# Second raw tiles for queries and keys in the first chunk of an attention and mixture kernel, with a new order of its steps

## The chip, the cores and the metric

The kernel runs on one core of one Trainium2 chip. The metric is the device time of one execution in microseconds (us), as the median of several runs. Engines are named as the profile names them: PE is TensorE, DVE is VectorE, ACT is ScalarE, POOL is GpSimd, and SP is the engine whose queue issues nearly all DMAs.

## The reference

What is computed, cut to what matters (4 batches, 8 heads, 576 positions, head size 64; then 2304 tokens of 512 features and 4 experts with 1024 hidden features, all float32):

```python
scores = (1 / sqrt(64)) * q @ k.T                      # per batch and head
thresh = max(scores) - tau                             # per row
scores = where(scores >= thresh, scores, -1e9)
attn = exp(scores - max(scores)); attn /= sum(attn) + 1e-9
x = attn @ v                                           # heads side by side: (2304, 512)
p = domain_probs / (sum(domain_probs) + 1e-9)          # (2304, 4)
for e in range(4):
    out += p[:, e:e+1] * (relu(x @ w1[e]) @ w2[e])
```

## The kernel before

**Values in two parts.** Products keep nearly full float32 precision by splitting a value into a rounded high part and a low remainder: ACT copies the raw tile to the high part (`q_hi`, `k_hi`, `v_hi`, `whi`, `hhi`), and DVE or POOL subtracts that from the raw tile for the low part (`q_lo`, `k_lo`, `v_lo`, `wlo`, `hlo`). One product is then two or three matmuls.

**Attention.** Two heads form a pair, and each head of a pair and a stretch of queries is a turn. Turns are counted through the kernel. A turn's transposed queries and keys are loaded into `q_raw` and `k_raw`, one tile each, from which the split parts go to tiles that alternate by turn (`q_hl`, `k_hh`, `k_ll`). A unit is 128 query rows of a pair (one unit may hold the end of the first head and the start of the second): `s` on PE makes its scores, then `max` (DVE, L991), `thr`, `exp` (ACT, L904), `mask` (DVE, L1002), `rec` (DVE), `norm` (POOL, L748), `tr` (PE transposes, L794), `phi` (ACT, L911 or L915) and, outside the first chunk, `plo` (DVE, L1014 and L1019) follow, and `pv` or `pv32` on PE multiplies by the values. `x_hi` (ACT) and `x_lo` (POOL) or `x_lo32` (DVE, L1031) split the result, which is the input of the experts.

**Chunks.** Tokens go in five chunks, of 384, 512, 384, 512 and 512. The first chunk has 4 pairs, 8 turns (0 to 7) of 384 queries and 24 units (`LONE` and `SOLID` are both 24). No expert works while they run, and so they may use a second score slot in the experts' PSUM tile `e_ps` (even units use `s_ps`, odd ones `e_ps`), and tiles named `solid` and a third `p` lie in SBUF where the experts' hidden tiles `h_hi` and `h_lo` are later. From unit 24 on units are interleaved with the experts of the chunk before; they have one score slot. The experts work in groups: `up` (PE, L848 to L850), whose result `hhi` (ACT, L940) and `hlo` (DVE, L1042) split, and `down` (PE, L863 to L865), whose result `acc` (DVE) adds up. Weights come in 320 pieces through a stage of 4 tiles into a ring of 14 (`w_load`, `whi` L950, `wlo` on POOL L760 or `wlo_dve` on DVE L1036). 16 pieces make an expert. Of the first expert pieces, those with m % 4 == 2 go to DVE.

**The order.** All engines walk one list, `ORDER`, and each picks its own steps from it, so each engine's instructions have a fixed order and only semaphores move them in time. `timeline()` gives every step a due time. A unit u of the first chunk starts at `first + period * u`, and each of its steps is due at an offset from the table `ALONE`; the later units have a start spread over the expert work and offsets from `AMONG`. The experts' start is `first + 24 * period + experts`. `settle()` then plays the steps through with a fixed duration for each. Whenever an engine is free in this model it takes, of the steps whose conditions in `follows()` are met, the one that is due first; steps of one kind keep their order; an SP step counts as landed 2.4 after its issue, which takes 1.2 (0.6 for a weight piece). Due times are thus priorities, not starting times.

**Loads.** For turn 1 and on, SP's `k_load` (L679) waits until `k_lo` of the turn before has read `k_raw` (`sp.wait_ge(s_klo, turn)`), and `q_load` (L671) until `q_lo` of the turn before has read `q_raw`. `v32_load` (L687, L689) and `v_load` (L695, L698) bring values, L709 weights. `k_lo` of turn 0 is on DVE (`k_lo_dve`, L977), all others on POOL (L733); `q_lo` is on DVE (L972).

Of the kernel before, what the change touches and what calls it, by code (L numbers as in the profile page):

```python
# [5 lines left out]
F32 = mybir.dt.float32  # L6
# [197 lines left out]
def ups_through(t, f):  # L204
# [7 lines left out]
ALONE = dict(load=-9.58, q_hi=6.24, q_lo=16.9, k_hi=3.19, k_lo=-5.05, v_hi=7.8, v_lo=-7.05, max=7.48, thr=16.58,  # L212
             exp=9.73, mask=14.89, eps=11.82, rec=0.41, norm=25.81, tr=-3.84, phi=12.87, plo=8.73, pv=18.85,
             xo=23.42, xs=7.11, x_hi=0.71, x_lo=7.48)
AMONG = dict(load=-9.73, q_hi=2.13, q_lo=6.73, k_hi=-6.56, k_lo=-8.85, v_hi=-5.72, v_lo=7.39, max=-2.85, thr=-2.6,
             exp=8.58, mask=2.91, eps=-2.89, rec=7.65, norm=-1.63, tr=10.81, phi=8.04, plo=-0.34, pv=12.11, xo=4.75,
             xs=15.23, x_hi=9.65, x_lo=8.74)
PLAN = dict(first=3.59, period=2.76, experts=17.92, end=13.35, weights=35.63, weight=8.82, prob=19.0)
# [144 lines left out]
def follows(name, x, half=2):  # L363
# [6 lines left out]
    if name == "k_load":  # L370
        return [(k_low(x - 1), x - 1)] if x else []
    if name in ("q_load", "v_load"):
        return [(name[0] + "_lo", x - 1)] if x else []
# [70 lines left out]
    return [("acc", x)]  # L444

# [80 lines left out]
def build(nc, qT, kT, v, tau, dp, w1, w2, out):  # L526
    ctx = ExitStack()
    with ctx:
# [28 lines left out]
        with nc.sbuf_tensor("solid", [P, FT, PAD], F32) as solid, nc.sbuf_tensor("p2", [P, PAD], F32) as p2:  # L557
            p.append(p2)
# [11 lines left out]
        e_ps = ctx.enter_context(nc.psum_tensor("e_ps", [P, 2, 512], F32))  # L570

# [13 lines left out]
        def head(turn):  # L585
            pair = PAIRS[turn // 2]
            return pair.b * H + 2 * pair.k + turn % 2

# [26 lines left out]
        s_q_ld = sem("s_q_ld")  # L615
        s_k_ld = sem("s_k_ld")
# [39 lines left out]
        TURNS32 = 2 * SOLID_PAIRS  # L656

        @block.sync
        def _(sp):
            sp.dma_start(tau_col[:, 0:1], tau.to_broadcast([P, 1])).then_inc(s_tau_ld, 16)  # L660
            for half in range(2):
                sp.dma_start(q_raw[half * HD:(half + 1) * HD, 0:PAIRS[0].n], qT[0][:, 0:PAIRS[0].n]).then_inc(s_q_ld, 16)
            for name, x in ORDER:
                if name == "q_load":
# [418 lines left out]
```

## Time and profile before

| | us |
|---|---|
| median of 3 runs (1089.19 to 1090.68) | 1090.0 |
| the profiled execution, its own time | 1088.7 |
| its span in the trace | 1086.7 |
| PE busy | 1061.0 (98%) |
| DVE busy | 674.6 (62%) |
| POOL busy | 629.0 (58%) |
| ACT busy | 562.2 (52%) |

The span is that of the profiled execution; its own time is 2.0 us longer, which lies around the span. Times in the trace are counted from the span's start. "Busy" is the time in which an engine executes an instruction; an idle time is put down to the one whose result came last. The granted clock of PE is at full speed in all 40 slices of the page. The chain that ended last is 92% PE, and the page has expert matmuls as its largest lines.

### The profile page before, as it was taken

The numbers are of one execution on the slowest core, as the hardware profiler recorded it, in microseconds if no ns is written. First come the engines' busy times: TensorE is split into PE (matmuls) and PEld (weight loads), VectorE is DVE, ScalarE is ACT, GpSimd is POOL, SyncE is SP. The second block draws the span as 40 slices with busy tenths as digits, with TensorE's granted clock in tenths as the row PEclk, the third lists the DMA queues.
The fourth block names the chain that finished last, engine by engine and source line by source line (L and its number), as shares of the span: only waits on it lengthen the run. The fifth ranks groups of instructions, "written<-read, shape, count | busy, mean of one in ns | idle before, by whom it ended". The sixth has DMA issues, their size and how long they took to land.

```text
span 1086.7 us, 17018 instructions
## 1 busy us (share of the span) xinstructions
PE 1061.0 (98%) x5752; PEld 931.5 (86%) x5752; DVE 674.6 (62%) x1505; ACT 562.2 (52%) x990; POOL 629.0 (58%) x659
## 2 busy tenths in 40 slices
PE   5899999999999999999999999999999999999998
PEld 5789899899888888888899999988888888888887
DVE  6988788787887788777777878752122133343331
ACT  6776566666766647566475656644233232242330
POOL 6756576767886748667486867656444342232220
PEclk9999999999999999999999999999999999999999
DMA  6534344445544424223333433333333244233311
GB/s 163 155 111 123 87 123 133 131 128 156 148 148 120 137 57 121 92 85 115 103 124 111 127 115 116 90 100 123 94 110 88 72 123 136 87 107 97 107 58 39
DMA packets 96788, 121.08 MB, mean 111 GB/s; under 512 B 41152, under 2 KB 45248, under 8 KB 96704
## 3 DMA queue, kind: packets, MB, share of 16 engines
q1 hardware_dynamic: 96400, 119.68, 37.0%
q8 instruction: 47, 0.77, 0.3%
q10 hardware_dynamic: 304, 0.33, 0.1%
q14 instruction: 37, 0.30, 0.1%
HBM read 115.25 MB, written 4.72 MB: 110 GB/s over the span
## 4 chain that ended last, share of the span: by engine, by line
PE 92%; DVE 4%; issue 1%; ACT 1%; POOL 1%; DMA 1%; SPq 0%; ACTq 0%; DVEq 0%
PE e_ps L863 12%; PE e_ps L865 12%; PE e_ps L864 12%; PE e_ps L848 12%; PE e_ps L850 12%; PE e_ps L849 12%; PE t_ps L794 6%; PE s_ps L782 3%; PE x_ps L821 3%; PE s_ps L783 3%; PE x_ps L823 3%; PE x_ps L806 1%; DVE p L1002 1%; DVE small L991 1%; DVE q_hl L972 0%
## 5 line engine op out<-in xcount | busy, mean ns | idle before, releaser
L760 POOL TENSOR_TENSOR w_lo<-stage,w_hi 128x512 fp32r<-128x512 f32 x272 | 355.8, 1319 | 275.6 <-ACT w_hi L950 275.3
L950 ACT ACTIVATE w_hi<-stage 128x512 fp32r<-128x512 f32 x320 | 194.1, 625 | 177.3 <-PE e_ps L865 120.6
L848 PE MATMUL e_ps<-x_hi,w_hi 128*128 128x512 f32 (+1 forms) x640 | 241.3, 377 | 0.2 <-DVE h_lo L1042 0.2
L850 PE MATMUL e_ps<-x_hi,w_lo 128*128 128x512 f32 (+1 forms) x640 | 236.2, 369 | 0.0
L849 PE MATMUL e_ps<-x_lo,w_hi 128*128 128x512 f32 (+1 forms) x640 | 235.8, 368 | 0.0
L863 PE MATMUL e_ps<-w_hi,h_hi 128*128 128x512 f32 x576 | 229.8, 399 | 0.0
L865 PE MATMUL e_ps<-w_hi,h_lo 128*128 128x512 f32 x576 | 225.2, 391 | 0.0
L864 PE MATMUL e_ps<-w_lo,h_hi 128*128 128x512 f32 x576 | 224.8, 390 | 0.0
L1042 DVE SCALAR_TENSOR_TENSOR h_lo<-e_ps,h_hi 128x512 fp32r<-128x512 f32 (+1 forms) x160 | 101.8, 636 | 127.1 <-ACT h_hi L940 125.1
L940 ACT ACTIVATE h_hi<-e_ps 128x512 fp32r<-128x512 f32 (+1 forms) x160 | 88.6, 554 | 118.0 <-PE e_ps L850 117.2
L904 ACT ACTIVATE p<-s_ps,small 128x576 f32<-128x576 f32 x132 | 97.4, 738 | 73.2 <-DVE small L991 72.7
L850 PEld LDWEIGHTS e_ps<-x_hi,w_lo 128*128 128x128 f32 x640 | 120.1, 188 | 15.6
L848 PEld LDWEIGHTS e_ps<-x_hi,w_hi 128*128 128x128 f32 x640 | 120.3, 188 | 13.7 <-DVE h_lo L1042 0.4
L849 PEld LDWEIGHTS e_ps<-x_lo,w_hi 128*128 128x128 f32 x640 | 120.4, 188 | 13.3
L865 PEld LDWEIGHTS e_ps<-w_hi,h_lo 128*128 128x128 f32 x576 | 108.1, 188 | 23.8
L864 PEld LDWEIGHTS e_ps<-w_lo,h_hi 128*128 128x128 f32 x576 | 108.4, 188 | 18.6
L1002 DVE SCALAR_TENSOR_TENSOR p<-s_ps,small,p 128x576 f32<-128x576 f32 x132 | 107.7, 816 | 26.4 <-ACT p L904 22.9
L863 PEld LDWEIGHTS e_ps<-w_hi,h_hi 128*128 128x128 f32 x576 | 108.3, 188 | 18.5
L748 POOL TENSOR_SCALAR p<-p,small 128x576 f32<-128x576 f32 x144 | 110.6, 769 | 22.9 <-DVE small L1009 11.5
L991 DVE TENSOR_REDUCE small<-s_ps 128x1 f32<-128x576 f32 x132 | 99.7, 756 | 34.2 <-PE s_ps L783 32.6
L915 ACT ACTIVATE pt_hi<-t_ps 128x640 fp32r<-128x640 f32 x120 | 84.4, 703 | 53.5 <-PE t_ps L794 52.2
L1059 DVE SCALAR_TENSOR_TENSOR acc<-e_ps,prob,acc 128x512 f32<-128x512 f32 x54 | 40.5, 750 | 111.2 <-PE e_ps L865 110.8
(64 smaller groups left out, 1465.0 us busy)
## 6 DMA issues: line engine op xcount, KB each, us to landing
stage<-w SPq DMA_DIRECT2D x320, 256.0 KB, 2.9
k_raw<-kT SPq DMA_DIRECT2D x94, 144.0 KB, 2.8
v_raw<-v SPq DMA_DIRECT2D x40, 128.0 KB, 2.2
out<-acc SPq DMA_DIRECT2D x18, 256.0 KB, 2.0
q_raw<-qT SPq DMA_DIRECT2D x32, 144.0 KB, 2.9
q_raw<-qT SPq DMA_DIRECT2D x16, 96.0 KB, 2.6
v_raw<-v SPq DMA_DIRECT2D x80, 16.0 KB, 2.1
q_raw<-qT SPq DMA_DIRECT2D x16, 80.0 KB, 2.4
```

The source lines that it names most:

```text
L748: gp.tensor_scalar(tile, tile, col(total, u), 1.0, ALU.mult, ALU.mult).then_inc(s_norm, 1)
L760: gp.tensor_tensor(w_lo[:, m % RING, :], stage[:, m % STAGES, :], w_hi[:, m % RING, :], ALU.subtract).then_inc(s_wl, 1)
L848: mm(ps[:, 0:n], w_hi[:, piece, tile], x_hi[:, k, cols], start=k == 0, stop=False)
L849: mm(ps[:, 0:n], w_hi[:, piece, tile], x_lo[:, k, cols], start=False, stop=False)
L850: op = mm(ps[:, 0:n], w_lo[:, piece, tile], x_hi[:, k, cols], start=False, stop=k == KT - 1)
L863: mm(ps, h_hi[:, f, tile], w_hi[:, piece, :], start=f == 0, stop=False)
L864: mm(ps, h_hi[:, f, tile], w_lo[:, piece, :], start=False, stop=False)
L865: op = mm(ps, h_lo[:, f, tile], w_hi[:, piece, :], start=False, stop=f == FT - 1)
L950: run(w_hi[:, m % RING, :], stage[:, m % STAGES, :], copy).then_inc(s_wh, 1)
L991: ve.tensor_reduce(col(neg_m, u), s_slot(u), AX.XY, ALU.max, negate=True).then_inc(s_max, 1)
L1002: ve.scalar_tensor_tensor(out=tile, in0=s_slot(u), scalar=col(thr, u), in1=tile, op0=ALU.is_ge, op1=ALU.mult, accum_out=col(total, u)).the ...
L1042: ve.scalar_tensor_tensor(out=h_lo[:, g.j, c0:c0 + n], in0=e_ps[:, g.bank, 0:n], scalar=0.0, in1=h_hi[:, g.j, c0:c0 + n], op0=ALU.max, op1 ...
```

## The change

For the 8 turns of the first chunk the raw queries and keys alternate between two tiles each: even turns keep `q_raw` and `k_raw`, odd turns use `q_raw2` (384 columns) and `k_raw2` (576 columns), which lie behind `solid` and the third `p` in the place of `h_hi` and `h_lo`. A load then waits for the low part of two turns before (`raw_before`); turn 8 follows turn 6, and from turn 9 on it is the turn before again. Each of the two load semaphores becomes a pair, one for even and one for odd turns. POOL's `k_lo` of turn 1 gets a wait for `k_lo` of turn 0, which is on DVE, so that the count of `s_klo` keeps its order. All due times are new (`ALONE`, `AMONG`, `PLAN`), and with them the order of all steps.

```diff
@@ -209,13 +209,13 @@
 
 
 
-ALONE = dict(load=-9.58, q_hi=6.24, q_lo=16.9, k_hi=3.19, k_lo=-5.05, v_hi=7.8, v_lo=-7.05, max=7.48, thr=16.58,
-             exp=9.73, mask=14.89, eps=11.82, rec=0.41, norm=25.81, tr=-3.84, phi=12.87, plo=8.73, pv=18.85,
-             xo=23.42, xs=7.11, x_hi=0.71, x_lo=7.48)
-AMONG = dict(load=-9.73, q_hi=2.13, q_lo=6.73, k_hi=-6.56, k_lo=-8.85, v_hi=-5.72, v_lo=7.39, max=-2.85, thr=-2.6,
-             exp=8.58, mask=2.91, eps=-2.89, rec=7.65, norm=-1.63, tr=10.81, phi=8.04, plo=-0.34, pv=12.11, xo=4.75,
-             xs=15.23, x_hi=9.65, x_lo=8.74)
-PLAN = dict(first=3.59, period=2.76, experts=17.92, end=13.35, weights=35.63, weight=8.82, prob=19.0)
+ALONE = dict(load=-11.01, q_hi=5.5, q_lo=23.24, k_hi=9.14, k_lo=-5.05, v_hi=7.26, v_lo=0.26, max=12.61, thr=24.24,
+             exp=16.27, mask=15.64, eps=1.79, rec=3.18, norm=27.13, tr=-0.14, phi=18.57, plo=6.84, pv=25.95,
+             xo=29.77, xs=12.98, x_hi=-1.84, x_lo=4.04)
+AMONG = dict(load=-4.47, q_hi=3.5, q_lo=7.9, k_hi=-3.85, k_lo=-2.77, v_hi=-4.59, v_lo=7.73, max=-4.35, thr=-4.57,
+             exp=8.78, mask=-0.65, eps=-0.09, rec=7.37, norm=2.02, tr=10.46, phi=7.72, plo=6.8, pv=12.14, xo=5.93,
+             xs=14.09, x_hi=9.71, x_lo=13.54)
+PLAN = dict(first=2.25, period=2.94, experts=17.27, end=13.3, weights=35.03, weight=9.15, prob=17.03)
 
 
 def halves_of(u):
@@ -368,8 +368,10 @@
     if name == "prob":
         return [("max", 4)]
     if name == "k_load":
-        return [(k_low(x - 1), x - 1)] if x else []
-    if name in ("q_load", "v_load"):
+        return [(k_low(raw_before(x)), raw_before(x))] if raw_before(x) >= 0 else []
+    if name == "q_load":
+        return [("q_lo", raw_before(x))] if raw_before(x) >= 0 else []
+    if name == "v_load":
         return [(name[0] + "_lo", x - 1)] if x else []
     if name == "v32_load":
         return [("pv32", last_unit(x - 2))] if x >= 2 else []
@@ -444,6 +446,11 @@
     return [("acc", x)]
 
 
+def raw_before(turn):
+
+    return turn - 2 if turn <= 2 * SOLID_PAIRS else turn - 1
+
+
 def k_low(turn):
 
     return "k_lo" if turn else "k_lo_dve"
...
-        with nc.sbuf_tensor("solid", [P, FT, PAD], F32) as solid, nc.sbuf_tensor("p2", [P, PAD], F32) as p2:
+
+        with (nc.sbuf_tensor("solid", [P, FT, PAD], F32) as solid, nc.sbuf_tensor("p2", [P, PAD], F32) as p2,
+              nc.sbuf_tensor("q_raw2", [P, PAIRS[0].n], F32) as q_raw2, nc.sbuf_tensor("k_raw2", [P, SEQ], F32) as k_raw2):
...
+        def q_in(turn):
+            return (q_raw2 if turn < TURNS32 and turn % 2 else q_raw)[:, 0:PAIRS[turn // 2].n]
+
+        def k_in(turn):
+            return k_raw2 if turn < TURNS32 and turn % 2 else k_raw
...
-        s_q_ld = sem("s_q_ld")
-        s_k_ld = sem("s_k_ld")
+        s_q_ld = [sem(f"s_q_ld{i}") for i in range(2)]
+        s_k_ld = [sem(f"s_k_ld{i}") for i in range(2)]
...
-                    sp.wait_ge(s_qlo, turn)
+                    if raw_before(turn) >= 0:
+                        sp.wait_ge(s_qlo, raw_before(turn) + 1)
                     for half in range(2):
-                        sp.dma_start(q_raw[half * HD:(half + 1) * HD, 0:pair.n],
-                                     qT[head(turn)][:, pair.q0:pair.q0 + pair.n]).then_inc(s_q_ld, 16)
+                        sp.dma_start(q_in(turn)[half * HD:(half + 1) * HD, :],
+                                     qT[head(turn)][:, pair.q0:pair.q0 + pair.n]).then_inc(s_q_ld[turn % 2], 16)
                 elif name == "k_load":
                     turn, = x
                     if turn == 0:
                         continue
-                    sp.wait_ge(s_klo, turn)
+                    if raw_before(turn) >= 0:
+                        sp.wait_ge(s_klo, raw_before(turn) + 1)
                     for half in range(2):
-                        sp.dma_start(k_raw[half * HD:(half + 1) * HD, :], kT[head(turn)]).then_inc(s_k_ld, 16)
+                        sp.dma_start(k_in(turn)[half * HD:(half + 1) * HD, :], kT[head(turn)]
+                                     ).then_inc(s_k_ld[turn % 2], 16)
...
-                    gp.tensor_tensor(k_ll[turn % 2][:], k_raw[:], k_hh[turn % 2][:], ALU.subtract).then_inc(s_klo, 1)
+                    if turn == 1:
+                        pool.wait_ge(s_klo, 1)
+                    gp.tensor_tensor(k_ll[turn % 2][:], k_in(turn)[:], k_hh[turn % 2][:], ALU.subtract).then_inc(s_klo, 1)
...
-                    act.wait_ge(s_q_ld, (turn + 1) * 32)
+                    act.wait_ge(s_q_ld[turn % 2], (turn // 2 + 1) * 32)
                     if turn >= 2:
                         act.wait_ge(s_s, last_unit(turn - 2) + 1)
-                    run(q_hl[turn % 2][:, q_cols(turn)], q_raw[:, 0:n], copy, scale=tau_col[:, 3:4]).then_inc(s_qhi, 1)
+                    run(q_hl[turn % 2][:, q_cols(turn)], q_in(turn), copy, scale=tau_col[:, 3:4]).then_inc(s_qhi, 1)
                 elif name == "k_hi":
                     turn, = x
-                    act.wait_ge(s_k_ld, (turn + 1) * 32)
+                    act.wait_ge(s_k_ld[turn % 2], (turn // 2 + 1) * 32)
                     if turn >= 2:
                         act.wait_ge(s_s, last_unit(turn - 2) + 1)
-                    run(k_hh[turn % 2][:], k_raw[:], copy).then_inc(s_khi, 1)
+                    run(k_hh[turn % 2][:], k_in(turn)[:], copy).then_inc(s_khi, 1)
```

`q_lo` and `k_lo_dve` read `q_in(turn)` and `k_in(turn)` in the same way; the first loads of turn 0 go to the same tiles as before.

## Rows read from the trace of the kernel before

**Rows 1.** The page's 40 equal slices of the span, busy tenths.
```profile
PE   5899999999999999999999999999999999999998
DVE  6988788787887788777777878752122133343331
```

**Rows 2.** Windows: each engine's busy us (instructions), clock, DMA share, GB/s.
```profile
9.16:83.06 73.90, 62.73 (x473) 58.10 (x473) 67.17 (x179) 53.57 (x89) 50.27 (x49) 1.00 0.49 141
...
83.06:1083.20 1000.14, 996.69 (x5277) 872.07 (x5275) 604.71 (x1319) 504.84 (x895) 575.27 (x598) 1.00 0.37 109
```

**Rows 3.** Waits of PE, 0 to 84 us: total, times, longest.
```profile
PE s_ps L782 <- DVE p L1002: 4.3, 4, 1.7
```

**Rows 4.** Waits of all engines, 0 to 95 us: the raw tiles' DMAs.
```profile
ACT k_hh L892 <- DMA k_raw<-kT: 1.6, 2, 1.2
...
ACT q_hl L886 <- DMA q_raw<-qT: 0.7, 1, 0.7
```

**Rows 5.** Timeline of SP's queue: start us, duration us, line, operation.
```profile
3.64 0.59 SPq L709 DMA_DIRECT2D stage<-w  x1
...
6.94 1.10 SPq L679 DMA_DIRECT2D k_raw<-kT  x2
```

**Rows 6.** Timeline of the engines, 10.5 to 16 us.
```profile
10.59 0.67 ACT L892 ACTIVATE k_hh<-k_raw 128x576 fp32r<-128x576 f32 x1
...
11.34 1.41 POOL L733 TENSOR_TENSOR k_ll<-k_raw,k_hh 128x576 fp32r<-128x576 f32 x1 [1.35 <-ACT k_hh L892]
12.73 0.75 POOL L748 TENSOR_SCALAR p<-p,small 128x576 f32<-128x576 f32 x1
...
11.83 0.17 DVE L1009 RECIPROCAL small<-small 128x1 f32<-128x1 f32 x1
11.93 0.82 DVE L1002 SCALAR_TENSOR_TENSOR p<-e_ps,small,p 128x576 f32<-128x576 f32 x1
...
14.19 0.62 DVE L972 SCALAR_TENSOR_TENSOR q_hl<-q_raw,small,q_hl 64x384 fp32r<-64x384 f32 x1
...
14.91 0.58 PE L782 MATMUL e_ps<-k_hh,q_hl 128*128 128x288 f32 x1
```

**Rows 7.** Timeline of ACT and DVE around 30 us.
```profile
29.79 0.61 ACT L886 ACTIVATE q_hl<-q_raw,small 128x384 fp32r<-128x384 f32 x1 [0.69 <-DMA q_raw<-qT]
...
31.66 0.82 DVE L1002 SCALAR_TENSOR_TENSOR p<-e_ps,small,p 128x576 f32<-128x576 f32 x1 [0.54 <-ACT p L904]
```

**Rows 8.** Timeline of ACT and DVE before the first expert matmul.
```profile
80.69 0.48 ACT L928 ACTIVATE x_hi<-x_ps 128x384 fp32r<-128x384 f32 x1
...
80.19 1.32 DVE L972 SCALAR_TENSOR_TENSOR q_hl<-q_raw,small,q_hl 64x192 fp32r<-64x192 f32 x1
...
82.29 0.55 DVE L1031 TENSOR_TENSOR x_lo<-x_ps,x_hi 128x384 fp32r<-128x384 f32 x1
```

**Rows 9.** Two lines over the whole span: min/median/max ns.
```profile
L1036 DVE TENSOR_TENSOR w_lo<-stage,w_hi x48: 672/693/1871, 17.7 to 1054.8; 128x512 fp32r<-128x512 f32 x48
...
L972 DVE SCALAR_TENSOR_TENSOR q_hl<-q_raw,small,q_hl x48: 418/919/1835, 6.9 to 675.4; 64x576 fp32r<-64x576 f32 x16, 64x384 fp32r<-64x384 f32 x8, 64x192 fp32r<-64x192 f32 x8, 64x320 fp32r<-64x320 f32 x8
```

**Rows 10.** Groups by line and shape, 0 to 85 us.
```profile
L1036 DVE TENSOR_TENSOR w_lo<-stage,w_hi 128x512 fp32r<-128x512 f32 x3 | 5.0, 1677 | 0.5 <-ACT w_hi L950 0.5
...
L972 DVE SCALAR_TENSOR_TENSOR q_hl<-q_raw,small,q_hl 64x192 fp32r<-64x192 f32 x3 | 3.4, 1141 | 0.2
```

**Rows 11.** Timeline of DVE and POOL around 57 us.
```profile
57.22 1.38 DVE L972 SCALAR_TENSOR_TENSOR q_hl<-q_raw,small,q_hl 64x384 fp32r<-64x384 f32 x1
...
56.76 1.43 POOL L733 TENSOR_TENSOR k_ll<-k_raw,k_hh 128x576 fp32r<-128x576 f32 x1 [1.11 <-ACT k_hh L892]
```

**Rows 12.** Timeline of DVE and PE around 206 us, expert stage.
```profile
202.27 0.76 DVE L991 TENSOR_REDUCE small<-s_ps 128x1 f32<-128x576 f32 x1
...
204.96 0.69 DVE L1014 TENSOR_TENSOR pt_lo<-t_ps,pt_hi 128x512 fp32r<-128x512 f32 x1
...
206.01 0.42 PE L821 MATMUL x_ps<-pt_hi,v_hl 128*128 128x320 f32 x1 [1.30 <-DVE pt_hi L1019]
```

More of the change, by code:

```diff
@@ L570, in build @@
         e_ps = ctx.enter_context(nc.psum_tensor("e_ps", [P, 2, 512], F32))
+        TURNS32 = 2 * SOLID_PAIRS
         def halves(ap):
@@ L655, in build @@
         ZEROS = 6
-        TURNS32 = 2 * SOLID_PAIRS
         @block.sync
@@ L661, in _ @@
             for half in range(2):
-                sp.dma_start(q_raw[half * HD:(half + 1) * HD, 0:PAIRS[0].n], qT[0][:, 0:PAIRS[0].n]).then_inc(s_q_ld, 16)
+                sp.dma_start(q_in(0)[half * HD:(half + 1) * HD, :], qT[0][:, 0:PAIRS[0].n]).then_inc(s_q_ld[0], 16)
             for name, x in ORDER:
@@ L872, in _ @@
             for half in range(2):
-                nc.scalar.dma_start(k_raw[half * HD:(half + 1) * HD, :], kT[0]).then_inc(s_k_ld, 16)
+                nc.scalar.dma_start(k_in(0)[half * HD:(half + 1) * HD, :], kT[0]).then_inc(s_k_ld[0], 16)
             nc.scalar.dma_start(dp_in, dp).then_inc(s_dp_ld, 16)
@@ L879, in _ @@
                     turn, = x
-                    n = PAIRS[turn // 2].n
                     if turn == 0:
                         act.wait_ge(s_tau, 5)
-                    act.wait_ge(s_q_ld, (turn + 1) * 32)
+                    act.wait_ge(s_q_ld[turn % 2], (turn // 2 + 1) * 32)
                     if turn >= 2:
                         act.wait_ge(s_s, last_unit(turn - 2) + 1)
-                    run(q_hl[turn % 2][:, q_cols(turn)], q_raw[:, 0:n], copy, scale=tau_col[:, 3:4]).then_inc(s_qhi, 1)
+                    run(q_hl[turn % 2][:, q_cols(turn)], q_in(turn), copy, scale=tau_col[:, 3:4]).then_inc(s_qhi, 1)
                 elif name == "k_hi":
                     turn, = x
-                    act.wait_ge(s_k_ld, (turn + 1) * 32)
+                    act.wait_ge(s_k_ld[turn % 2], (turn // 2 + 1) * 32)
                     if turn >= 2:
                         act.wait_ge(s_s, last_unit(turn - 2) + 1)
-                    run(k_hh[turn % 2][:], k_raw[:], copy).then_inc(s_khi, 1)
+                    run(k_hh[turn % 2][:], k_in(turn)[:], copy).then_inc(s_khi, 1)
                 elif name == "v_hi":
@@ L968, in _ @@
                     turn, = x
-                    n = PAIRS[turn // 2].n
                     dve.wait_ge(s_qhi, turn + 1)
                     lo = q_hl[turn % 2][HD:P, q_cols(turn)]
-                    ve.scalar_tensor_tensor(out=lo, in0=q_raw[HD:P, 0:n], scalar=tau_col[HD:P, 3:4],
+                    ve.scalar_tensor_tensor(out=lo, in0=q_in(turn)[HD:P, :], scalar=tau_col[HD:P, 3:4],
                                             in1=lo.bitcast(F32), op0=ALU.mult, op1=ALU.subtract).then_inc(s_qlo, 1)
@@ L976, in _ @@
                     dve.wait_ge(s_khi, turn + 1)
-                    ve.tensor_tensor(k_ll[turn % 2][:], k_raw[:], k_hh[turn % 2][:], ALU.subtract).then_inc(s_klo, 1)
+                    ve.tensor_tensor(k_ll[turn % 2][:], k_in(turn)[:], k_hh[turn % 2][:], ALU.subtract).then_inc(s_klo, 1)
                 elif name == "prob":
```

## The prediction

> **What bounds the kernel now.** The page comes first: TensorE (PE) shows a 9 in every slice of 27 us but the first two and the last, and VectorE (DVE) reaches its own 9 in the second slice and falls in the last third [rows 1]. The second and third slice are where PE may have a rival, so there are two stages to tell apart. The table of windows puts a number on them. From 83.06 us, where the first expert matmul starts, to 1083.20, where the last ends, PE is busy 996.69 of 1000.14 us: only 3.45 us are idle, and the order can give back no more than that. From 9.16 us, where DVE takes its first maximum, to 83.06 DVE is busy 67.17 of 73.90 us and PE 62.73 [rows 2]. Here DVE is the bound, and its 6.73 us of idle time is what a better order could save, before any change in the length of its instructions. The last 3.5 us of the span (1086.7 - 1083.2) are the final sum and store and stay. The waits of that first stage are the next view: besides the start, before the first scores, PE waits most for DVE's masks (4.3 us), that is, for DVE to free a score slot [rows 3]. The waits for the raw tiles' DMAs are small: 1.6 us for keys, of which 1.2 is the very first load, and 0.7 us for queries [rows 4]. So the second raw tile attacks about 1.1 us of direct waiting and whatever hangs on the order of the loads.
>
> **The change part by part, against the profiled execution (1088.7 us).**
>
> *Start.* I work out the order from the planner's own rules; its internal clock serves for the order alone, the times are the trace's. In the old order SP issues after v32_load(0) a weight piece and v_load(8), since k_load(1) must wait for k_lo(0): k_load(1) goes out at 6.94, q_load(1) behind it [rows 5]. The old rules, gone through by hand, give this order. With raw_before(1) < 0, k_load(1) is free as soon as k_load(0) has landed in the planner, is due at 2.25 + 3 x 2.94 - 11.01 = 0.1, and so takes the weight piece's place at 3.64; q_load(1) follows at about 4.8, then v32_load(1), k_load(2), q_load(2), and only then the weight and v_load(8), at about 9.6. Keys of turn 1 are then rounded by ACT near 7.6 to 8.3 instead of at 10.59, and k_lo(1) leaves POOL near 9.7 instead of 12.75 [rows 6]. What this releases: the first norm stood behind k_lo(1) at 12.73, while its reciprocal was ready at 12.00 (11.83 + 0.16), so it starts 0.7 us sooner, and q_lo(1), which ended at 14.81 and held the scores of unit 3 until 14.91, is done some 3 us earlier. Unit 3's other condition, the mask of unit 1, ended at 12.75 (11.93 + 0.82), and a transpose may still stand before it, so its scores start between 0 and 2.1 us earlier; I take 0.8, one transpose short of the full gain. The 0.7 us of q_lo(1) moves out of this stretch into idle DVE time partly: 0.3 more. Together -1.1 us, bounds -2.1 and 0. The moved weight and value loads lie about 6 us later; the weight pieces are asked for only at 83.06, and v_load(8) at the end of the stage, so this costs nothing. Should weights be late after all, one POOL low part is 1.3 us.
>
> *Steady stretch of the first stage.* Each turn lasts three units. Only one place shows the single query tile deciding: q_hi at 29.79 waited 0.69 us for its load, which puts ACT's following steps back, and DVE then stands 0.54 us before the mask at 31.66 [rows 7]. With two tiles the load is free one turn earlier. DVE being the bound, the gain is its idle time: -0.5, bounds -0.8 and 0. The other six turns show no raw wait; their gain is zero.
>
> *End of the first stage.* The last x_lo32 starts on DVE at 82.29 though its x_hi started on ACT at 80.69 and took 0.48: ahead of it stand q_lo(10) with 1.32 and a mask [rows 8]. In the new numbers x_hi is due 2.6 us sooner and x_lo32 3.4 us sooner relative to its unit, and the loads of the second chunk are due later (-9.73 to -4.47). The planner's availability decides too, so I count about two thirds of the 1.1 us (82.29 - 81.17): -0.8, bounds -1.6 (x_hi stood behind ACT work as well) and +0.8.
>
> *New order in the expert stage.* All PE work there is the same, with 3.45 us of idle [rows 2]. The largest piece is 1.30 us at 206.01: its pt_lo started on DVE only at 204.96, after a run of other DVE work that began with the maximum at 202.27 [rows 12]. I take 0, bounds -2 and +5 (below).
>
> *Tiles, semaphores and the new wait.* q_raw2 and k_raw2 lie in h's place. h_hi is first written after the first expert matmuls, and the second pair's last readers, q_lo(7) and k_lo(7), precede the last scores of the first chunk; no wait, no cost. POOL's new wait in k_lo(1) is for k_lo(0) on DVE, after which the old k_load(1) went out at 6.94 [rows 5], so it is over before any k_lo(1) can start; behind it stands only later POOL work: 0.
>
> *Length of DVE instructions.* Three w_lo in the first stage take 1677 ns on average against a least of 672 over the kernel, three short q_lo 1141 against 418 [rows 9, 10]. That is 3 x 1.00 + 3 x 0.72 = 5.2 us. The long q_lo at 57.22 took 1.38 us and ended (58.60) 0.41 us after POOL's k_ll (56.76 + 1.43 = 58.19) [rows 11], while that at 14.19 took 0.62 [rows 6]: it stood while the other engine worked. A new order redraws these meetings; I take 0, bounds -4 and +3.
>
> The Trainium skill (SBUF - State Buffer, "Who interferes with whom") says that a VectorE instruction with both inputs in SBUF and a GpSimd one that reads SBUF exclude each other: the second waits for the whole of the first. The pair at 57.22 agrees. By this rule earlier k_lo and q_lo could just as well meet more often, as the planner prices neither; its extreme is the rival on meetings below.
>
> Sum: 1088.7 - 1.1 - 0.5 - 0.8 = 1086.3. The profiled execution lies 1.3 below the median of the three timed runs (1090.0), so in the terms of the median: **1087.6**.
>
> **The rivals.**
> 1. *The first stage stays DVE-bound and the gains are swallowed.* For it: 67.17 of 73.90 us busy, raw waits of 1.1 us after the start. Against it: the start is a dependent chain, where DVE does wait. Time: start -0.5, the rest 0: 1089.5.
> 2. *Fewer meetings of DVE and POOL.* For it: 5.2 us of DVE time is lengthening [rows 9, 10] in the stage where DVE is the bound. Against: nothing in the change aims at it. Half of it on top of the forecast, 2.6: 1085.0.
> 3. *Slower: pt_lo loses its place in the expert stage.* AMONG's plo goes from -0.34 to 6.8 and max from -2.85 to -4.35. The planner starts units some 5 us apart there (the first chunk: (133 us of expert work in its own costs - 13) / 32 units + 1.7 = 5.4), so the maximum of two units later is due at 10 - 2.85 = 7.2 (old, after plo) and 10 - 4.35 = 5.7 (new, before plo). pt_lo frees the transposes' PSUM tile and the pv matmuls; PE executes in a fixed order, so it stands. Price: one stall like that at 206.01, 1.3 us, of which the old trace has one, for 120 units that need a pt_lo (the code's count). It decides from the fourth further stall on: four cost 5.2 and turn 1087.6 into 1092.8. Against it: PE waits three times in 1000 us, so the order has reserve, and the planner places the PE work after its model of DVE.
> 4. *The changed order does nothing at the start* (k_load(1) still issued late): in rival 1.
>
> **How the numbers follow.** Forecast 0.50 (own range 1086.0 to 1089.4), rival 1 0.18, rival 2 0.12, rival 3 0.20. A change of 0.2% (2.2 us) is about what a measurement of this kernel can tell from none. The forecast is 2.4 below, near that bound, but its unknown terms are open further downwards (-4) than up inside the first stage: I give 0.36 of its 0.50 to faster and 0.14 to same. Faster 0.36 + 0.12 = 0.48; same 0.14 + 0.18 = 0.32; slower 0.20. Range: down to 1084.0 (rival 2 with two thirds of the lengthening gone, 3.6), up to 1092.0, which leaves out rival 3's far part.
>
> **What would show it.** k_raw's second load issued before 5 us; the scores of unit 3 before 14.5; the first expert matmul near 80.7 instead of 83.06; PE's idle time from there to the end still 3 to 4 us. Wrong if the first expert matmul does not move (rival 1), if w_lo and q_lo of the first stage have a different mean length (rival 2 or its opposite), or if PE waits for L1014 and L1019 in the expert stage (rival 3).

## The result: 1094.1 us against 1091.2, slower where faster was forecast

| | before | changed |
|---|---|---|
| median of 22 runs each, us | 1091.16 (1089.19 to 1094.94) | 1094.07 (1091.14 to 1095.54) |
| the profiled execution, its own time | 1088.7 | 1094.13 |
| its span | 1086.7 | 1092.2 |

The ratio is 1.002, 95% interval 1.0013 to 1.0028. A second set (e9 below, 10 runs of the changed kernel, 33 of the one before) gave 1.0029 (1.0015 to 1.0043). The kernel became slower by some 2 to 3 us; the forecast was 1087.6, and the range ended at 1092.0.

The page of the changed kernel has the same shape as [rows 1]:

```profile
span 1092.2 us, 17019 instructions
...
PE 1063.6 (97%) x5752; PEld 932.8 (85%) x5752; DVE 672.4 (62%) x1505; ACT 562.4 (51%) x990; POOL 628.7 (58%) x659
...
PE   5898999999999999999999999999999999999998
...
DVE  6888687888787878878787878762122133343331
```

The table of windows (engines in the order of the page, then granted clock, DMA share, GB/s) stands against [rows 2]:

```profile
9.16:85.37 76.21, 62.96 (x474) 58.55 (x474) 64.80 (x179) 53.48 (x90) 50.13 (x49) 1.00 0.48 135
85.37:88.80 3.43, 3.43 (x14) 3.43 (x13) 2.97 (x9) 1.08 (x2) 1.07 (x2) 0.52 0.39 104
88.80:1088.70 999.90, 995.81 (x5265) 869.66 (x5263) 601.92 (x1311) 503.89 (x893) 574.66 (x596) 1.00 0.37 109
```

The first expert matmul starts at 85.37 instead of 83.06: +2.31. Directly behind it the mean granted clock is 0.52 for 3.43 us: nearly all of that stretch is at the lower of its two levels, 1.2 instead of 2.4 GHz. PE's timeline shows what that is:

```profile
84.74 0.40 PE L803 MATMUL s_ps<-k_hh,q_hl 128*128 128x288 f32 x1 [2.92 <-DVE p L1021]
...
85.91 0.52 PE L871 MATMUL e_ps<-x_hi,w_lo 128*128 128x384 f32 x1
86.23 0.52 PE L869 MATMUL e_ps<-x_hi,w_hi 128*128 128x384 f32 x1
...
89.19 0.34 PE L870 MATMUL e_ps<-x_lo,w_hi 128*128 128x384 f32 x1
89.36 0.33 PE L871 MATMUL e_ps<-x_hi,w_lo 128*128 128x384 f32 x1
```

PE stood 2.92 us for a mask before the scores that come just ahead of the experts; then one expert matmul follows another every 0.32 us instead of every 0.17. The twelve steps from 85.37 to 89.01 take 3.64 us, and at 0.174 each, as behind 89.01, they would take 2.09: the fall of the clock costs 1.55. From the first to the last expert matmul it is 1003.33 us against 1000.14, +3.19; without the 1.55 some 1.6 remain. So the span's 5.5 is 2.31 + 1.55 + 1.64. The medians differ only by 2.9, so part of the 5.5 belongs to these two executions and not to the kernels; the experiments tell which.

The forecast's first signs came as written. Against [rows 5, 6], SP's queue, ACT and POOL at the start:

```profile
3.65 1.24 SPq L697 DMA_DIRECT2D k_raw<-kT  x2
4.93 1.24 SPq L688 DMA_DIRECT2D q_raw<-qT  x2
...
9.95 0.58 SPq L728 DMA_DIRECT2D stage<-w  x1
```

```profile
7.82 0.68 ACT L912 ACTIVATE k_hh<-k_raw 128x576 fp32r<-128x576 f32 x1 [1.11 <-DMA k_raw<-kT]
...
8.58 1.43 POOL L754 TENSOR_TENSOR k_ll<-k_raw,k_hh 128x576 fp32r<-128x576 f32 x1 [5.73 <-ACT k_hh L912]
```

Keys of turn 1 are loaded 3.3 us sooner and their low part is 2.76 us sooner. The scores of unit 3 start at 13.73 instead of 14.91, a gain of 1.18, before the 14.5 that the forecast gave as a sign. But DVE then does something that the forecast did not have:

```profile
11.07 0.62 DVE L991 SCALAR_TENSOR_TENSOR q_hl<-q_raw,small,q_hl 64x384 fp32r<-64x384 f32 x1
11.72 0.82 DVE L1021 SCALAR_TENSOR_TENSOR p<-s_ps,small,p 128x576 f32<-128x576 f32 x1
...
15.13 1.11 DVE L991 SCALAR_TENSOR_TENSOR q_hl<-q_raw,small,q_hl 64x384 fp32r<-64x384 f32 x1
```

`q_lo(1)` at 11.07, three microseconds sooner as forecast, now stands ahead of the first mask, which starts at 11.72 where it was 10.79; `q_lo(2)` at 15.13 stands ahead of the maximum of unit 3, and the mask of unit 2 starts at 17.05 where it was 15.07.

### The profile page after: what moved, and what is told of

Same layout as the page of the kernel before. It is cut to its first block, busy times and chain, and to the rows that moved or that the text cites. A ratio compares the mean times of both kernels' runs of the same rounds, so it can differ in the third digit from the quotient of the medians.

```text
span 1092.2 us, 17019 instructions
## 1 busy us (share of the span) xinstructions
PE 1063.6 (97%) x5752; PEld 932.8 (85%) x5752; DVE 672.4 (62%) x1505; ACT 562.4 (51%) x990; POOL 628.7 (58%) x659
## 4 chain that ended last, share of the span: by engine, by line
PE 90%; DVE 3%; issue 2%; POOL 1%; DMA 1%; ACT 1%; SPq 1%; ACTq 0%; DVEq 0%
PE e_ps L869 12%; PE e_ps L871 12%; PE e_ps L870 12%; PE e_ps L884 12%; PE e_ps L886 11%; PE e_ps L885 11%; PE t_ps L815 7%; PE s_ps L803 3%; PE s_ps L804 3%; PE x_ps L842 3%; PE x_ps L844 2%; PE x_ps L827 1%; DMA stage<-w 1%; DVE p L1021 1%; POOL w_lo L781 1%
## 5 line engine op out<-in xcount | busy, mean ns | idle before, releaser
L1010 DVE TENSOR_REDUCE small<-s_ps 128x1 f32<-128x576 f32 x132 | 99.7, 756 | 38.0 <-PE s_ps L804 36.7
L815 PE MATMUL t_ps<-ident,p 128*128 128x128 f32 x720 | 103.8, 275 | 6.5 <-ACT solid L931 4.1
```

Source lines behind the costliest of these rows:

```text
L815: op = nc.tensor.transpose(t_ps[:, tile], p[p_slot(u)][:, tile], ident[:])
```

## The experiments

Each was timed beside the kernel before on one chip: e1 to e4 on a first (29 runs of the kernel before), e5 to e8 on a second (35), e9 to e12 on a third (33). "First up" is the start of the first expert matmul, "expert" the time from there to the end of the last matmul, both of the profiled execution ([rows 2] stop 0.23 us before that end). In the last column is its mean granted clock over the span: 1.0, or 0.998 where the clock was at the lower level once, for 3.4 us (0.997: twice).

| run | median (n) | ratio [95%] | first up | expert | clock |
|---|---|---|---|---|---|
| before, first profile | 1091.16 (22) | | 83.06 | 1000.37 | 1.0 |
| changed, first profile | 1094.07 (22) | 1.002 [1.0013, 1.0028] | 85.37 | 1003.56 | .998 |
| e1 tiles, old order | 1090.87 (12) | 0.9989 [0.9979, 1.0] | 83.12 | 1000.52 | 1.0 |
| e2 tiles and rule, old numbers | 1099.19 (6) | 1.0064 [1.0048, 1.008] | 86.58 | 1007.71 | .997 |
| e3 new numbers, one tile | 1092.15 (12) | 1.0004 [0.9995, 1.0013] | 84.92 | 1003.35 | .998 |
| e4 end's steps moved | 1093.62 (12) | 1.002 [1.0008, 1.0032] | 85.95 | 1005.05 | .998 |
| e5 new order in the first stage only | 1091.43 (12) | 1.0006 [0.9993, 1.0019] | 86.28 | 1000.45 | .998 |
| e6 turn 9 on the second tile | 1091.7 (12) | 1.0003 [0.9991, 1.0016] | 86.47 | 1001.79 | .998 |
| e7 start's steps put back | 1091.94 (12) | 1.0011 [0.9999, 1.0024] | 83.72 | 1001.57 | 1.0 |
| e8 old order, last x_lo32 first | 1090.96 (12) | 1.0002 [0.9991, 1.0012] | 84.56 | 1003.69 | .998 |
| e9 the changed kernel again | 1094.02 (10) | 1.0029 [1.0015, 1.0043] | 84.57 | 1002.19 | 1.0 |
| e10 new order in the expert stage only | 1092.37 (11) | 1.0009 [1.0, 1.0017] | 83.80 | 1002.0 | 1.0 |
| e11 as e5 | 1091.8 (12) | 1.0 [0.9989, 1.001] | 87.42 | 1000.63 | .998 |
| e12 as e1 | 1090.46 (12) | 0.9992 [0.9982, 1.0001] | 84.67 | 1000.34 | .998 |

The place of the fall matters for "first up". It began at 31.6 to 33.9 us in the profiles of e3, e4, e5, e6, e8, e11 and e12, at 85.5 in the first profile of the changed kernel, and at 43.3 and 214.0 in e2. A profile with a fall near 32 us has its whole cost in "first up": e1 and e12 are the same kernel, and e12, with the fall, is 1.55 later there. So such a profile is set below against others that have one.

**e1 to e4: tiles or order?** e1 keeps the second tiles, their waits and semaphores, and takes every number and the old load rule of the planner back, so that all steps stand in the old order:

```diff
-        return [(k_low(raw_before(x)), raw_before(x))] if raw_before(x) >= 0 else []
+        return [(k_low(x - 1), x - 1)] if x else []      # in the planner alone; q_load likewise
-ALONE = dict(load=-11.01, q_hi=5.5, q_lo=23.24, ...
+ALONE = dict(load=-9.58, q_hi=6.24, q_lo=16.9, ...       # AMONG and PLAN likewise
```

> The second raw tiles and their laxer waits, with every engine's order exactly as in the kernel before. Theory 'order' (the time is lost by the changed order, the tiles are harmless): within 0.1% of before, ratio 0.999 to 1.001, first expert matmul within 0.5 us of 83.06, granted clock 1.0 throughout. Theory 'tiles' (a load that lands earlier disturbs something, a port or a DMA): ratio 1.001 to 1.003, first expert matmul 1 us or more later.

Measured 1090.87 against 1091.64, 0.9989. The tiles cost nothing, and the interval just touches 1. The profile is at full clock, as expected; 9 of the 12 executions are not.

e2 takes only the numbers back (the last two lines above) and leaves the looser load rule in.

> The second raw tiles with the planner knowing of them, but all due times of the kernel before. Theory 'numbers' (the new due times lose the time): ratio 0.998 to 1.0005. Theory 'laxer loads' (being allowed to load early is what reorders the first stage for the worse): ratio 1.001 to 1.003, first expert matmul 1 to 2.5 us later than 83.06.

Measured 1099.19, 1.0064: the worst of all, and beyond the range of either theory. Freeing the loads in the planner while the due times are old moves 272 of PE's 976 steps, and both stages lose (first up 86.58, expert 1007.71, each with one fall of the clock in it). In the windows, PE gets less done in the same stretch than in e1:

```profile
9.16:83.00 73.84, 58.98 (x442) 54.36 (x442) 61.68 (x173) 50.03 (x84) 47.74 (x48) 0.98 0.49 139
```

```profile
9.16:83.00 73.84, 63.01 (x474) 58.51 (x474) 65.55 (x179) 53.40 (x89) 50.18 (x49) 1.00 0.50 138
```

The first row is e2 with 442 matmuls, the second e1 with 474. The new numbers thus repair most of what the looser rule does, but not all.

e3 is the other half: all new numbers, but one raw tile and the old rule.

```diff
-            return k_raw2 if turn < TURNS32 and turn % 2 else k_raw
+            return k_raw                             # q_in likewise; one semaphore each
```

> The new due times with the single raw tiles of the kernel before. Theory 'numbers': as slow as the changed kernel or slower, ratio 1.002 to 1.004. Theory 'laxer loads': close to before, 0.999 to 1.001.

Measured 1.0004, not told from 1 by itself. With the old rule in the planner these numbers do not give the order of the changed kernel: by the list of steps e3 has the order of e10 below, step for step, in which PE's first stage stands as before. So e3 tests the new expert order, not the new numbers in the first stage.

e4 tests the end of the first stage, where the forecast had its -0.8: on top of the change, the second chunk's steps go behind the last split of x.

```diff
+put_after([("k_hi", (10,)), ("q_hi", (10,))], ("x_hi", (PAIRS[3],)))
+put_after([("q_lo", (10,))], ("x_lo32", (PAIRS[3],)))
```

> The changed kernel with k_hi(10), q_hi(10) and q_lo(10) moved behind x_hi of pair 3 and x_lo32 of pair 3, so that the end of the first chunk no longer stands behind the load of turn 10. Theory 'end of the stage' (ACT's wait of 1.6 us for turn 10's keys delays x_hi(3), PE stands 2.9 us, and its clock falls to half for 3.4 us): first expert matmul near 83, PE idle before it under 2 us, granted clock 1.0 there, time 3 to 4 us below the changed kernel, ratio to before 0.998 to 1.000. Theory 'body' (the time was lost before 75 us or in the expert stage): at most 1 us gained, ratio 1.001 to 1.003.

Measured 1093.62, 1.002, as slow as the changed kernel. The edit did what it should: from the start of the last mask of the chunk to the first expert matmul it was 7.54 us against 9.64 in the first profile of the changed kernel (8.46 in its second, e9) and 9.59 before. But the stage behind took it back; PE's waits there are new:

```profile
85.31 0.40 PE L816 MATMUL s_ps<-k_hh,q_hl 128*128 128x288 f32 x1 [0.81 <-DVE p L1034]
...
90.60 0.77 PE L828 MATMUL t_ps<-ident,p 128*128 128x128 f32 x5 [1.36 <-POOL p L782]
```

The transposes wait for the norm of unit 25, the second of the second chunk, and that waited for its reciprocal (L1041) on DVE, behind the very step that had been moved:

```profile
85.76 1.32 DVE L1004 SCALAR_TENSOR_TENSOR q_hl<-q_raw,small,q_hl 64x192 fp32r<-64x192 f32 x1
```

```profile
89.39 0.32 POOL L780 TENSOR_SCALAR p<-p,small 128x64 f32<-128x64 f32 x1 [2.52 <-DVE small L1041]
```

The keys were not late here: their low part was on POOL at 85.43. Expert was 1005.05.

**e5 to e8: which stage, and which place in it?** e5 takes only `AMONG` back. Of PE's 976 steps in the order 43 stand elsewhere than in the kernel before, all in the first stage.

```diff
-AMONG = dict(load=-4.47, q_hi=3.5, q_lo=7.9, ...
+AMONG = dict(load=-9.73, q_hi=2.13, q_lo=6.73, ...
```

> The changed kernel with the old AMONG numbers. By the list of steps its expert stage is then in the order of the kernel before, step for step, and its first stage in that of the changed kernel: 43 of 976 PE steps differ from before, all in the first stage. Theory 'first stage' (the new order of the first chunk loses the time): first expert matmul at 85.4 plus or minus 0.3, ratio 1.0015 to 1.003. Theory 'expert stage' (the 108 reordered PE steps after it lose it): ratio below 1.001.

Measured 1.0006, below the 1.001 that 'expert stage' asked for, and expert is back at 1000.45. The interval, to 1.0019, does not by itself tell it from the changed kernel.

e6 lets turn 9 use the second tile too, with the order untouched, against the wait for `k_raw` at 80 us that the first profile showed.

```diff
-    return turn - 2 if turn <= 2 * SOLID_PAIRS else turn - 1
+    return turn - 2 if turn <= 10 else turn - 1      # in SP's waits alone; tiles to match
```

> The changed kernel, order untouched, but turn 9 also uses the second raw tiles, so that the loads of turn 10 wait for the low parts of turn 8 and not of turn 9. Theory 'turn 10's load' (the end of the stage hangs on q_load(10), k_load(10) and ACT's wait of 1.6 us for them): that wait is gone, first expert matmul near 83.8, 1.6 us earlier than in the changed kernel, PE idle before it 1.3 instead of 2.9 us, ratio to before 1.000 to 1.0015. Theory 'scores late' (something else is right behind): first expert matmul moves by under 0.5 us.

Measured 1.0003. ACT no longer waited for the tenth turn's keys, but first up came at 86.47. With the fall near 32 us it belongs beside e5 (86.28) and e11 (87.42), whose first stage has the same order and no such tile: nothing shows that the wait had set it. The time came out 2.4 us lower than for the changed kernel (1091.70 against 1094.07 and 1094.02), and this profile does not explain it. The changed kernel was not timed on this chip, so the chip is a rival that was not tested. Beside e5, which lacks only the new expert order and the ninth turn's tile, e6 is 0.3 us slower, where the square below finds 2.2 for that order. The intervals of e6 (to 1.0016) and of the changed kernel (from 1.0013) just overlap.

e7 puts back the two placements at the start:

```diff
+put_after([("q_lo", (1,))], ("mask", (1,)))
+put_after([("s", (3,))], ("tr", (0, 2)))
```

> The changed kernel with q_lo(1) behind mask(1) on DVE and the scores of unit 3 behind the transposes of unit 0 on PE, as before. The first mask starts near 10.8 instead of 11.7. Theory 'the start decides': the first expert matmul moves by the same 0.9 us or more. Theory 'the start is absorbed' (masks 4 to 10 of the changed kernel are level with before in spite of it): first expert matmul within 0.4 us of 85.4, ratio as the changed kernel, 1.0015 to 1.003.

Measured 1.0011 [0.9999, 1.0024]. The first mask was back at 10.76, and the masks of units 4 to 10 came 1.1 to 2.4 us sooner than in the kernel before. By unit 17 that lead was gone (0.7 later than before), and first up was 83.72: the stage swallowed a gain at its start, as rival 1 says. Against the changed kernel the edit did move the end of the stage: 1.65 earlier than in its first profile, and 0.85 earlier than in e9 (84.57), which like e7 is at full clock. That is what 'the start decides' asked for, so about half of e9's delay of 1.51 may hang on these two placements. What it is worth in the kernel's time is not shown: e7 is 2.1 us below the changed kernel, timed elsewhere, but 0.2 above e6 on the same chip.

e8 tries the end on the old order:

```diff
+put_after([("q_lo", (10,))], ("x_lo32", (PAIRS[3],)))
+put_after([("s", (26,))], ("up", (GROUPS[0], 0)))
```

> The second raw tiles with the order of the kernel before, but q_lo(10) behind x_lo32 of pair 3 on DVE and the scores of unit 26 behind the first half of the first expert group on PE. Theory 'the end of the stage is worth having' (the term of the prediction that the new order did not bring): first expert matmul near 82.2, 0.9 us earlier than 83.1, and that much off the time, ratio 0.9975 to 0.9995. Theory 'given back' (the gain returns as a wait of the next units): the first expert matmul is earlier but the span is not shorter than that of the tiles with the old order, 1086.9.

Measured 1.0002, beside 0.9989 for the same tiles without it. From the last mask of the chunk to first up it was 6.90 us against 9.58 in e1 and e12, but the last mask itself came 2.6 us later than in e12, for which the edit gives no reason, so that first up (84.56) is level with e12's. PE again waited for a norm just behind (1.5 us at 90.18), and expert was 1003.69, 3.3 more than in e12.

**e9 to e12: the square.** The last four cross the two stages on one chip. e9 is the changed kernel, e11 is e5, e12 is e1. e10 has all new numbers with the old load rule in the planner; by this the first stage keeps the old order but for one swap of a turn's two copies on ACT and one of two loads on SP, and 108 of PE's steps differ, none before the 130th.

```diff
-        return [(k_low(raw_before(x)), raw_before(x))] if raw_before(x) >= 0 else []
+        return [(k_low(x - 1), x - 1)] if x else []      # in the planner alone; q_load likewise
```

> The changed kernel once more, as one corner of a square whose four corners run on one chip: both stages in the new order. Theory 'two orders add' (first stage about +1.0 us, expert stage about +1.4 us): ratio 1.0015 to 1.003, and the sum of the excesses of the two corners with one new order each. Theory 'one profile's accident' (turn 10's keys landing 3.5 us after their issue, which only that profile had): in this profile ACT does not wait for them, and the first expert matmul is near 84 where the clock holds, 86 where it fell in the first stage.

Measured 1.0029; first up 84.57 at full clock, and ACT did not wait for those keys. What was expected of the sum is answered below.

> Second raw tiles, first stage in the old order, expert stage in the new one (all new due times, without the looser load rule in the planner: 108 of 976 PE steps differ from before, all behind step 130). Theory 'expert order loses' : from first expert matmul to the last PE instruction 1001.5 to 1002 us without a fall of the clock in it, against 1000.4 before; ratio 1.001 to 1.0015. Theory 'it is all in the first stage': 1000.4 and ratio below 1.0005.

Measured 1.0009 [1.0, 1.0017], between the two theories, with expert 1002.00 and no fall, as 'expert order loses' has it.

> Second raw tiles, first stage in the new order, expert stage in the old one, on the same chip as the other corners. Theory 'two orders add': first expert matmul near 84 where the clock holds (before 83.06), 86.3 where it fell; the rest 1000.4; ratio 1.0005 to 1.0015. Theory 'it is all in the first stage': ratio as the changed kernel.

Measured 1.0000 [0.9989, 1.001], below the range of 'two orders add'; expert 1000.63; first up 87.42, with the fall, 1.1 later than expected.

> Second raw tiles, both stages in the old order, on the same chip as the other corners. If the tiles alone gain nothing, ratio 0.9995 to 1.0005; if the 0.1% of their first run holds, 0.998 to 0.9995. First expert matmul 83.1, rest 1000.4 to 1000.5.

Measured 0.9992 [0.9982, 1.0001], expert 1000.34; first up 84.67, with a fall at 32.2.

| median, us | old expert order | new expert order |
|---|---|---|
| old first stage | 1090.46 (e12) | 1092.37 (e10) |
| new first stage | 1091.80 (e11) | 1094.02 (e9) |

The new expert order costs 1.91 and 2.22, the new first stage 1.34 and 1.65. Drawing the 10 to 12 executions of each corner again at random, many times over, gives an interval (95%) of 0.5 to 2.7 for the 1.91 and 0.2 to 5.5 for the 2.22, so the expert order's cost is shown in both rows; it gives -0.7 to 2.5 and -0.1 to 4.5 for the first stage, whose cost is not. 1.34 + 1.91 = 3.25 is near the 3.56 for both, but that the two add is not shown: the difference of 0.31 has an interval of -1.9 to 3.9, and by the ratios to the kernel before the corners are 1.0009, 1.0000 and 1.0029. The tiles themselves cost nothing.

The two profiles at full clock, before and e9, say the same of their executions: e9's span is 3.3 us longer (1090.0 against 1086.7), 1.51 up to first up and 1.82 behind it.

**Where the expert order loses.** Every profile with the old expert order untouched has expert 1000.34 to 1000.63 (before, e1, e5, e11, e12). With the new one it is 1001.57 to 1002.19 (e6, e7, e9, e10, and the changed kernel less its 1.55), and 1003.35 in e3, with one tile. At some points both orders have the same steps of PE behind them, so that their times can be compared. Us behind the kernel before, counted from each one's first up, at five such points:

| before's time | e10 | e9 | e7 | e6 | e3 | e12 (old order) |
|---|---|---|---|---|---|---|
| 151.4 | -0.10 | -0.34 | -0.34 | -0.44 | -0.36 | -0.07 |
| 203.4 | 1.40 | 1.26 | 0.80 | 0.91 | 2.09 | -0.12 |
| 250.0 | -0.22 | -0.40 | -0.81 | -0.67 | 0.40 | -0.12 |
| 284.1 | 1.66 | 1.91 | 1.25 | 1.27 | 3.08 | 0.09 |
| 1060.1 | 1.64 | 1.82 | 1.21 | 1.43 | 2.99 | -0.02 |

The new order loses between 151 and 203, wins most or all of that back by 231, where the stall of 1.30 [rows 12] is gone, and loses it for good between 250 and 284; behind that little changes. Mean durations of PE's matmuls by shape are equal to 1.5 ns. The difference is in waits, and the weight loads' row shows it more fully than the matmuls', whose ends are modelled. Waits of the weight loads from 86 to 345 us, first e12 (old order), then e10 (new):

```profile
PEld x_ps L840 <- DVE pt_hi L1036: 1.9, 2, 1.6
PEld s_ps L801 <- DVE p L1019: 0.9, 2, 0.5
PEld t_ps L813 <- POOL p L767: 0.6, 2, 0.4
PEld e_ps L867 <- DVE h_lo L1059: 0.4, 1, 0.4
```

```profile
PEld s_ps L801 <- DVE p L1019: 1.9, 3, 0.9
PEld t_ps L813 <- issue: 1.7, 3, 0.9
PEld t_ps L813 <- POOL p L767: 1.5, 4, 0.5
PEld x_ps L840 <- DVE pt_hi L1036: 1.1, 3, 0.4
PEld e_ps L867 <- DVE h_lo L1059: 0.2, 1, 0.2
```

3.8 us in 7 waits against 6.4 in 14. One long stall went, that of 1.30 us at 206 [rows 12], and a handful of short ones came, of half a microsecond or less. In the stretch that decides, 250 to 290 us, e12 has one wait of the weight loads, 0.4 us for a norm, and e10 has five:

```profile
PEld t_ps L813 <- POOL p L767: 1.0, 2, 0.5
PEld s_ps L801 <- DVE p L1019: 0.7, 1, 0.7
PEld t_ps L813 <- issue: 0.6, 1, 0.6
PEld x_ps L840 <- DVE pt_hi L1036: 0.4, 1, 0.4
```

Four of the stalls as PE's own row has them in e10, two before 203 us and two in that stretch:

```profile
161.78 0.40 PE L801 MATMUL s_ps<-k_hh,q_hl 128*128 128x288 f32 x1 [0.50 <-DVE p L1019]
...
164.43 0.74 PE L813 MATMUL t_ps<-ident,p 128*128 128x128 f32 x5 [0.47 <-DVE pt_hi L1036]
...
256.71 0.40 PE L801 MATMUL s_ps<-k_hh,q_hl 128*128 128x288 f32 x1 [0.41 <-DVE p L1019]
...
285.98 0.74 PE L813 MATMUL t_ps<-ident,p 128*128 128x128 f32 x5 [0.22 <-DVE pt_hi L1036]
```

The second and the fourth wait for `plo`, which reads the transposes' PSUM tile; the first and the third wait for masks.

**What the first stage and the clock do together.** For each execution but the first 22 of the kernel before its mean granted clock is known. Medians by whether it stayed at full speed throughout (n) or not (n), all runs of one order taken together:

| order | clock at full speed | clock fell |
|---|---|---|
| before | 1090.08 (23) | 1091.63 (74) |
| tiles, old order (e1, e12) | 1089.43 (6) | 1091.14 (18) |
| first stage new (e5, e11) | 1089.18 (7) | 1092.07 (17) |
| expert stage new (e3, e10) | 1091.43 (9) | 1092.49 (14) |
| both new (changed, e9) | 1091.95 (4) | 1094.24 (28) |

Beside the tiles in the old order the expert order costs 2.0 us at full clock and 1.35 with a fall. By these medians the first stage costs nothing at full clock (1089.18 against 1089.43) and 0.9 with a fall. That its loss lies in executions in which the clock fell is a guess: drawn again at random the two differences run from -1.5 to 1.4 and from -0.1 to 1.9, the groups come from different chips, and e9's profile, at full clock, has first up 1.51 later than before, where e10, with the old first stage, has 0.74 and e1 0.06. With a fall near 32 us it is 86.28 to 87.42 with the new first stage (e5, e6, e11) against 84.67 and 84.92 with the old one (e12, e3). How often the clock falls also differs by set: in 28 of 29, 23 of 35 and 23 of 33 executions of the kernel before. A fall in e11's first stage, PE alone (window, busy, granted clock, DMA share, GB/s):

```profile
30.00:31.00 1.00, 0.75 (x5) 1.00 0.68 206
31.00:32.00 1.00, 0.20 (x2) 1.00 0.76 229
32.00:33.00 1.00, 1.00 (x8) 0.74 0.41 95
33.00:34.00 1.00, 1.00 (x7) 0.50 0.25 51
34.00:35.00 1.00, 1.00 (x6) 0.50 0.12 21
35.00:36.00 1.00, 1.00 (x7) 0.55 0.68 217
36.00:37.00 1.00, 1.00 (x10) 1.00 0.80 305
```

PE had waited 0.80 us for a norm until 30.25, and waited 0.80 for ACT's copy of the transposes until 31.81; then it was busy throughout, at half clock for 3.4 us. The Trainium skill (TensorE: Matmul & The Clock Gate, "HAM oscillation — how this bites in real kernels") says that idle gaps of PE throttle it again and that the work behind them runs cold. The rows here agree in kind, though its example has longer gaps than the two of 0.80: 0.74 and 0.50 follow a microsecond in which PE was busy for 0.20. They do not tell when it happens: the same kernel (e9 and the changed one) ran both with and without a fall, and the kernel before has gaps of up to 1.7 us [rows 3] in a profile without one.

## Why the prediction was wrong

- **Start, -1.1: the load order was right, the sum was not.** SP issued as worked out, `k_lo(1)` came 2.76 us sooner, and the scores of unit 3 came 1.18 sooner (0.8 was counted). The step that failed is that this was carried to the end of the stage, and that "q_lo(1) ... is done some 3 us earlier" was counted as gain alone. DVE's order was not worked out: with q_lo free early, the planner put it ahead of the first mask (+0.93). Putting it back (e7) made the masks of units 4 to 10 earlier than before by 1.1 to 2.4 us; at the end of the stage 0.85 was left against the changed kernel's e9, and first up was still 0.66 later than before.
- **Steady, -0.5: the wait was misread.** "Only one place shows the single query tile deciding", says the forecast of the 0.69 at 29.79 [rows 7]. In e1, with two tiles and the old order, the same wait is there:

```profile
30.37 0.61 ACT L904 ACTIVATE q_hl<-q_raw,small 128x384 fp32r<-128x384 f32 x1 [0.73 <-DMA q_raw<-qT]
```

The load stands in SP's order behind a value load and a key load, and goes out right behind them, at 27.12 (26.57 before): SP's order decided, not the tile. In the changed kernel the wait went, and DVE ran through 31 us without a stop, but the stage ended no sooner.
- **End, -0.8: no such move.** On ACT and DVE the last steps of the first chunk stand in the same order in both kernels. The argument by due times could not hold: by the old numbers x_lo32 was already due at 74.55 and q_lo(10) at 111.07, so the order that the forecast wanted was the preferred one before, and availability decided. And "2.6 us sooner ... relative to its unit" leaves out that the unit itself is due 2.8 later. e4 and e8 forced the move, the end of the stage became 2.1 us (0.9 against e9) and 2.7 us shorter, and the next stage gave it back. So this term was zero twice over.
- **Expert stage, 0 with bounds -2 and +5: mis-sized, and the likeliest part of the loss.** The step that failed is its 0: it was +1.6 in the first profile, +1.9 and +2.2 in the square. The argument from 3.45 us of idle time, that "the order can give back no more", bounded the gain and said nothing of the loss, which has no such bound. The sign that was to warn, PE's idle time of 3 to 4 us, was 4.1 in the first profile: a modelled busy time hides most of such a loss. The rows were misread too: the longest wait of PE in that stage is not the 1.30 at 206.01 but one of 1.47 at 443.68, for a mask, and it stands unchanged in e10; and PE waits five times there, not three.
- **Rival 3 had the sign and the stage, and the mechanism only in part.** Waits for pt_lo did come up, but at 0.5 us or less each in e10, not 1.3, and beside more waits for masks and norms. The two numbers it named are not the cause either: in the planner's order, taking plo alone to 6.8 on the old numbers, or max alone to -4.35, moves no PE step. The numbers act together.
- **Length of DVE's instructions, 0: the term moved and bought nothing.** The three w_lo took 831 ns on average instead of 1677 [rows 10]:

```profile
L991 DVE SCALAR_TENSOR_TENSOR q_hl<-q_raw,small,q_hl 64x192 fp32r<-64x192 f32 x3 | 3.5, 1165 | 1.4 <-ACT q_hl L906 1.3
...
L1055 DVE TENSOR_TENSOR w_lo<-stage,w_hi 128x512 fp32r<-128x512 f32 x3 | 2.5, 831 | 0.0
```

DVE's busy time to the first expert matmul fell by 2.4 us (64.80 from 67.17) while the stage grew by 2.3: its idle time went from 6.7 to 11.4. This is the deeper error: I read 67.17 busy of 73.90 as "DVE is the bound". e1 shows it without any change of order: its three w_lo take 1046 ns on average, DVE is busy 65.67 of the 73.96 us to first up, 1.5 less than before, and first up is 83.12 against 83.06. Rival 2 fell with it. What is left, that the stage is a chain through DVE, ACT, POOL and PE and is long where one of them waits for another, is my reading of the waits and not tested.
- **The base.** The profiled execution before was one in which the clock never fell, as in only 23 of the 97 later executions of that kernel, and its median over more runs is 1091.2, not the 1090.0 of the first three. That is 1.2 us of the miss of 6.5 (1094.1 - 1087.6). The rest: 2.4 of forecast gain that did not come, and 2.9 of loss: 1.2 + 2.4 + 2.9 = 6.5.
- **Of the first profile's +5.5,** some is that execution's own. Its late start of the experts and its half clock at 85 us are not in e9, the same kernel: first up 84.57, clock 1.0, and no wait for keys; e9's span is 3.3 us above before's. In the first profile those keys were asked for at 76.75, and ACT could begin with them only at 81.45:

```profile
75.60 1.11 SPq L688 DMA_DIRECT2D q_raw<-qT  x2
76.75 1.24 SPq L697 DMA_DIRECT2D k_raw<-kT  x2
```

```profile
81.45 0.68 ACT L912 ACTIVATE k_hh<-k_raw 128x576 fp32r<-128x576 f32 x1 [1.61 <-DMA k_raw<-kT]
```

What stays open: whether the new order of the first stage costs time in the median, and by what path it loses the 1.5 us of e9's profile; why e6, with both new orders, came out at 1.0003; and which single displaced step starts the short stalls between 250 and 284 us. The planner itself is no guide: in its own model the changed order starts its last step 0.56 us sooner than the old one (1143.69 against 1144.25), and on the chip it is 2.9 later.

**A version that may be ahead of both** is the second tiles with the old order: 0.9989 and 0.9992 in two sets of 12 runs, about 1 us. Each interval ends at or just above 1, so the gain is not shown.

## What to carry to other kernels

A change of one wait in a kernel with a planned order is two changes, the wait and the new order, and the second can be the larger: run the wait with the old order first (e1), and cross the stages when the whole doesn't equal the parts. Where PE is busy 99.7% of a stage, a new order has nearly nothing to win there and more to lose. Look for the loss at points where both orders have the same work behind them: stalls that one part of a stage loses and the next wins back say nothing of the end. A high busy share of an engine in a stage made of chains names no bound; ask whether the stage shortens when that engine's work does.

## What was not expected of the hardware

In 74 of 97 executions of the kernel before, on one core and with PE busy 98% of its profiled execution, TensorE's mean granted clock was below 1.0; in 65 of them it was 0.998, which is what one stretch of 3.4 us at the lower level makes of 1087 us. Nine of the fourteen profiles have such a stretch, and in seven of them it began between 31 and 34 us, in the old order of the first stage as in the new. A fall is worth 1.6 us (1091.63 against 1090.08), more than any term of the forecast, and a single profile of either kind misplaces the median by about as much. And the keys' load of one kernel, issued at the same place, took 3.5 us from the end of its issue (76.75 + 1.24 = 77.99) to ACT's start at 81.45 in one execution, and had landed before ACT asked for it in another.
